# Transposing the last expert slot on TensorE, and spreading the next block's sums and squares over successive steps

## What is computed

```python
# experts: top 2 of 8, N=3072 tokens, D=384, F=1024
h = np.maximum(x[mask] @ w1[e], 0.0)
out[mask] += top2_w[mask, k, None] * (h @ w2[e])
# output network, d_ff=1536
rms = np.sqrt(np.mean(x * x, axis=-1, keepdims=True) + 1e-06)
xn = x / rms * rms_g
g = xn @ w_gate
silu = g * (1.0 / (1.0 + np.exp(-g)))
return (silu * (xn @ w_val) @ w_out)
```

## Time and profile before

| What | us |
|---|---|
| median of three runs | 1308.37 |
| the profiled execution | 1309.53 |
| its span, first to last instruction | 1307.8 |
| attention, up to about | 300 |
| experts, up to the last output matmul | 814.4 |
| first matmul of the output network | 832.5 |
| PE busy | 1244.2 (95%) |
| DVE busy | 858.9 (66%) |
| ACT busy | 458.4 (35%) |

### The profile page before, as it was taken

One profiled execution on the slowest core, in us unless ns is written; L12 is line 12 of the kernel. 1 busy time (PEld: TensorE's weight loads), 2 busy tenths in 40 slices (PEclk: granted clock), 3 DMA queues, 4 the chain that ended last, 5 costly groups with the idle time before them and its releaser, 6 DMA issues.

```text
span 1307.8 us, 26515 instructions
## 1 busy us (share of the span) xinstructions
PE 1244.2 (95%) x8915; PEld 1143.2 (87%) x8916; DVE 858.9 (66%) x1941; ACT 458.4 (35%) x982; POOL 444.2 (34%) x374
## 2 busy tenths in 40 slices
PE   4999999999899999999999998699999999999998
PEld 4777878777789989899998987599999999999997
DVE  7898888876578778787877876344454444444433
ACT  3565665654232222223222222233232323233221
POOL 8467777734641606061455530311010101010000
PEclk9999999999999999999999999699999999999999
DMA  5233433245413222232314310211010101010000
GB/s 214 87 97 127 131 124 119 65 165 224 145 50 133 84 99 99 85 113 73 132 48 161 140 43 25 73 37 37 19 55 1 55 19 37 19 36 18 0 19 19
DMA packets 36175, 105.46 MB, mean 81 GB/s; under 512 B 4992, under 2 KB 20352, under 8 KB 33664
## 3 DMA queue, kind: packets, MB, share of 16 engines
q1 hardware_dynamic: 27504, 56.41, 12.9%
q0 software_dynamic: 8592, 47.98, 10.3%
HBM read 77.83 MB, written 26.54 MB: 80 GB/s over the span
## 4 chain that ended last, share of the span: by engine, by line
PE 75%; DVE 7%; POOL 6%; issue 5%; ACT 5%; DMA 2%; another core or an unknown queue 0%; DVEq 0%; SPq 0%; ACTq 0%; POOLq 0%
PE pD L1776 12%; PE pD L1885 9%; PE pA L1885 9%; PE pA L1808 9%; PE pS L1808 8%; PE pA L1899 6%; PE pA L1584 5%; PE pA L1776 5%; PE pS L1899 3%; PE pA L1790 2%; PE pX L1749 1%; POOL qk L583 1%; DVE W L1087 1%; POOL prods L599 1%; DMA stage<-w 1%
## 5 line engine op out<-in xcount | busy, mean ns | idle before, releaser
L1520 DVE TENSOR_TENSOR gs<-pD,sig 128x384 f32<-128x384 f32 x96 | 53.5, 557 | 200.3 <-ACT sig L1022 200.3
L1263 DVE STREAM_TRANSPOSE pA<-pD 32x128 f32<-32x128 f32 x416 | 138.1, 332 | 54.6 <-PE pD L1776 48.9
L751 POOL DMA_INDIRECT pair<-y_sorted,y_row x48 | 46.5, 968 | 342.9 <-DVE z L1499 272.5
L1263 DVE STREAM_TRANSPOSE pA<-pA 32x128 f32<-32x128 f32 x400 | 132.8, 332 | 43.6 <-PE pA L1776 38.0
L926 ACT ACTIVATE hidH<-pA 128x512 fp32r<-128x512 f32 x110 | 65.8, 600 | 254.5 <-DVE pA L1263 244.9
L1584 PE MATMUL pA<-W 64*128 64x128 f32 (+3 forms) x1920 | 138.0, 284 | 16.3 <-DVE W L1087 13.0
L1776 PE MATMUL pD<-we,xsH 128*128 x462 | 145.6, 396 | 0.0
L1584 PEld LDWEIGHTS pA<-W 64*128 64x128 f32 (+3 forms) x1920 | 113.8, 171 | 35.5 <-DVE W L1087 18.7
L1022 ACT ACTIVATE sig<-pD 128x384 f32<-128x384 f32 x96 | 47.1, 491 | 211.2 <-PE pA L1885 211.1
L1808 PE MATMUL pA<-we,hidH 128*128 (+1 forms) x464 | 120.9, 342 | 0.0
L1087 DVE TENSOR_TENSOR W<-W,prods 128x512 f32<-128x512 f32 (+1 forms) x120 | 102.7, 862 | 20.9 <-PE pA L1584 17.1
(11 more groups left out here) (262 smaller groups left out, 2875.2 us busy)
## 6 DMA issues: line engine op xcount, KB each, us to landing
stage<-w POOLq DMA_DIRECT2D x14, 1536.0 KB
qk<-qk_t SPq DMA_DIRECT2D x24, 512.0 KB, 3.8
xs<-x_sorted SPq DMA_DIRECT2D x55, 192.0 KB, 2.4
y_sorted<-yo SPq DMA_DIRECT2D x55, 192.0 KB, 1.9
fT<-f_t SPq DMA_DIRECT2D x12, 512.0 KB, 5.7
vN<-v_n SPq DMA_DIRECT2D x24, 256.0 KB, 2.6
out<-fin SPq DMA_DIRECT2D x8, 576.0 KB, 2.8
stage<-w SPq DMA_DIRECT2D x2, 1536.0 KB
```

Source lines behind the costliest of these rows:

```text
L751: pool.indirect_dma_start(out=pair[:, j, k], out_offset=None, in_=y_sorted[:, :], in_offset=bass.IndirectOffsetOnAxis(ap=y_row[:, t * TS + ...
L1263: ins = dve.transpose(by_32[1][32 * q:32 * (q + 1), :, i], by_32[0][32 * i:32 * (i + 1), :, q])
L1520: dve.tensor_tensor(gs[:], pD[:, f % 2 * 512:f % 2 * 512 + TT], sig[f % 2][:], ALU.mult).then_inc(s_u, 1)
```

## The change

Two parts that have nothing to do with each other.

The last slot (`last_slot(t)`, t = 54): ACT rectifies both halves, PE transposes both (lines 1790 and 1795), and DVE's 16 transposes fall away. ACT's rectifying of the second half waits for the end of hidden(54), and PE's transposes wait for both rectified halves.

The output stage: `combine` becomes one call for each tile, at f = 2, 3 and 4, with its own semaphore steps; the squares are taken one tile each at f = 3, 4 and 5; the root stands at f = 6 alone; `norm` moves from f = 6 to f = 7. Semaphore `s_z` now counts 8 a block and `s_ms` 4. POOL's gathers wait for the third tile's sum.

```diff
+        def last_slot(t):
+            return t.i is None and t.c == SLOTS - 1
-        ZS, ZS_PAIR = 5, 2
+        ZS, MS = 8, 4
@@ POOL
-                    pool.wait_ge(s_z, (t - 2) * ZS + ZS_PAIR)
+                    pool.wait_ge(s_z, (t - 2) * ZS + 2 * TS)
@@ ACT rectify
-                if early(t):
+                if last_slot(t):
+                    act.wait_ge(s_ht, SLOTS - 1)
+                if early(t) or last_slot(t):
                     act.wait_ge(s_g1, t.times(2, 2))
                     ins = act.activation(hid[:, HF:], hidden_bank(t, 1), ACT.Relu)
@@ ACT
-            def mean_square(t):
+            def square_of(t, j):
+                act.wait_ge(s_z, t.times(ZS, 2 * j + 2 - ZS))
+                act.activation(square[j][:], z[:, j], ACT.Square, accum_out=ms[:, j:j + 1]).then_inc(s_ms, 1)
+            def root(t):
+                act.wait_ge(s_ms, t.times(MS, TS - MS))
                 if t.c >= 2:
-                    act.wait_ge(s_z, t.times(ZS, -2 - ZS))
+                    act.wait_ge(s_z, t.times(ZS, -1 - ZS))
                 act.activation(rms[:], ms[:], ACT.Sqrt, scale=1.0 / DM, bias=eps[:]).then_inc(s_ms, 1)
@@ ACT wide
-                    if f == 4 and (t + 1).before(NT2):
-                        mean_square(t + 1)
+                    if NEXT_SUM < f <= NEXT_SUM + TS and (t + 1).before(NT2):
+                        square_of(t + 1, f - NEXT_SUM - 1)
+                    if f == NEXT_SUM + TS + 1 and (t + 1).before(NT2):
+                        root(t + 1)
@@ DVE turn_hidden
+                if last_slot(t):
+                    return
@@ DVE
-            def combine(t):
-                for s in s_pair:
-                    dve.wait_ge(s, t.times(32, 32))
+            def combine(t, j):
+                dve.wait_ge(s_pair[j], t.times(32, 32))
@@ DVE wide
-                    if f == 3 and more:
-                        combine(t + 1)
-                    if f == 6 and more:
+                    if NEXT_SUM <= f < NEXT_SUM + TS and more:
+                        combine(t + 1, f - NEXT_SUM)
+                    if f == NEXT_Z - 1 and more:
                         norm(t + 1)
@@ PE turn_hidden
-                    pe.wait_ge(s_hl, t.times(2, 0 if early(t) else -1))
+                    pe.wait_ge(s_hl, t.times(2, 0 if early(t) or last_slot(t) else -1))
-                if early(t):
+                if early(t) or last_slot(t):
                     for k in range(FC // 2):
```

More of the change, by code:

```diff
@@ L460, in clear_rows @@
                 eng.dma_start(x_sorted[bass.ds(n + e * REGION, P), :], zero[:]).then_inc(s_zero, 16)
-        NEXT_Z = 8
+        NEXT_SUM, NEXT_Z = 2, 8
         TAB_COUNT, TAB = 1, 16
-        ZS, ZS_PAIR = 5, 2
+        ZS, MS = 8, 4
         FIRST_SUM, FIRST_NORM = (2, 4, 8), (6, 10, 12)
@@ L998, in first_mean_square @@
                                bias=eps[:]).then_inc(s_rms, 1)
-            def mean_square(t):
-                act.wait_ge(s_z, t.times(ZS, ZS_PAIR - ZS))
-                if t.c >= 2:
-                    act.wait_ge(s_z, t.times(ZS, -2 - ZS))
[L1005 to L1008, removed]
+            def square_of(t, j):
[3 more added lines that the diff above has]
+                act.wait_ge(s_ms, t.times(MS, TS - MS))
+                if t.c >= 2:
+                    act.wait_ge(s_z, t.times(ZS, -1 - ZS))
                 act.activation(rms[:], ms[:], ACT.Sqrt, scale=1.0 / DM, bias=eps[:]).then_inc(s_ms, 1)
@@ L1485, in first_norm @@
                 dve.tensor_scalar(z[:, j], z[:, j], inv[:, j:j + 1], None, ALU.mult).then_inc(s_first, 1)
-            def combine(t):
-                for s in s_pair:
-                    dve.wait_ge(s, t.times(32, 32))
[L1491 to L1501, removed]
+            def combine(t, j):
+                dve.wait_ge(s_pair[j], t.times(32, 32))
+                if j == 0:
+                    dve.wait_ge(s_tz, t.times(KC))
+                sh = share[:, bass.ds(t.times(TS, j), 1)]
+                dve.tensor_scalar(z[:, j], pair[:, j, 0], sh[:, 0, 0:1], None, ALU.mult).then_inc(s_z, 1)
+                dve.wait_ge(s_z, t.times(ZS, 2 * j + 1 - ZS))
+                dve.scalar_tensor_tensor(out=z[:, j], in0=pair[:, j, 1], scalar=sh[:, 0, 1:2], in1=z[:, j],
+                                         op0=ALU.mult, op1=ALU.add).then_inc(s_z, 1)
             def norm(t):
-                dve.wait_ge(s_ms, t.times(2))
+                dve.wait_ge(s_ms, t.times(MS))
                 dve.reciprocal(inv[:], rms[:]).then_inc(s_z, 1)
-                dve.wait_ge(s_z, t.times(ZS, 3 - ZS))
+                dve.wait_ge(s_z, t.times(ZS, 2 * TS + 1 - ZS))
                 for j in range(TS):
                     ins = dve.tensor_scalar(z[:, j], z[:, j], inv[:, j:j + 1], None, ALU.mult)
-                ins.then_inc(s_z, 2)
+                ins.then_inc(s_z, 1)
             def low_z(t, k):
```

## The result

The changed kernel takes 1302.0 us, the median of 9 runs from 1300.65 to 1305.37; the kernel before, 9 runs beside it, 1308.37 (1305.15 to 1309.28). The ratio over all these runs, which is not that of the two medians (0.9951), is 0.9964 with a 95% interval of 0.9951 to 0.9977. Two more comparisons in later sessions gave 0.9954 (0.9941 to 0.9968) and 0.9954 (0.9940 to 0.9967). So the change makes the kernel 0.4 to 0.5% faster, some 5 to 6 us. The kernel before took between 1303.7 and 1308.4 us in the four sessions, the last three of them on three different chips, so whole times are set side by side only within a session.

A forecast was written before the change was run, and what follows sets the result against it. PE was taken to bound the output stage, and the path through output(54) everything up to the output network. 1309.53 - 2.4 - 4.4 = 1302.7 us, less 0.4 for the median: 1302.3, between 1300.3 and 1304.3 (1300.0 to 1305.3 with rivals).

The forecast's parts named there:

- part 1: Last slot: output(54) starts 0.80 us earlier and runs at full clock, saving 1.58 more; -2.4 us in all.
- part 2: Output stage: seven stops of PE for `uL` fall away, with their refill and restart; -4.4 us.
- Seven stops: Output stage: PE's waits for `uL`, 2.6 us idle together plus 0.16 and 0.10 each, all to go; -4.4 us.
- the sigmoid of step 6 starts at T + 3.84: Output stage, T being the start of its gate_value: the sigmoid starts at T + 3.84 instead of T + 3.46, 0.38 late.
- the 1.2 us to spare: Output stage: margin left before PE stops, with the sigmoid of step 6 0.38 us late against 1.60 allowed.
- the allowance of 1.60: Output stage: a sigmoid may start 1.60 us late before PE feels it, from 2.22 less 0.62.
- the way to output(53): Last slot: stop of 0.69 us and transposes of 0.50 and 0.35 put output(53)'s first matmul at 803.32, 1.35 us later.
- the clock's 1.58 us: Last slot: output(54) took 5.66 us at the lower clock against 4.08 for output(53); 1.58 us to be saved.
- Rival 1: Last slot: the clock falls all the same, costing 1.58 us again; 1304.3 us, chance 0.12.
- Rival 2: Output stage: half its stops stay, from a longer table exchange or sums that push a product; 1304.9 us, chance 0.10.
- Rival 4: Either part does hardly anything, as the stop moves on to something unseen; 1305 to 1308 us, chance 0.08.
- Rival 3: Output stage: table exchange takes 5.46 us, the sigmoid of step 6 is 2.94 late, PE stops; 1312.8 us, chance 0.04.

The follow-up runs named there:

- experiment 3: Changed kernel with an extra, unread root and sigmoid of 128x3 ahead of the root; 1320.0 us, against 1301.87 of the changed kernel beside it.
- experiment 2: Changed kernel with the three sums and the three squares each all at once again, only the root apart; 1298.02 us, 0.9960 of the kernel before.
- experiment 5: Changed kernel with the last slot's second half transposed behind output(53), halves signalled singly; 1297.27 and 1299.07 us, 0.9954 and 0.9956 of the kernel before.
- part 1 alone: Kernel before with only the last slot changed, output stage as before; 1303.19 and 1306.65 us in two sessions, 0.9997 and 0.9993 of the kernel before.

## Why the prediction was right, point by point

**The total.** 1302.3 was forecast, 1302.0 measured. That they lie so close is in part luck: the nine runs of the changed kernel lie 4.7 us apart, the last 0.4 us of the forecast were a guess, and part 1 was put too high and part 2 a little too low. The sum was made for the profiled execution, and 6.8 us were to go from it; 7.3 went from the span behind the first matmul of the experts. The medians fell by 6.4, 6.0 and 6.6 us in three comparisons, the ratios say 4.7 to 6.

**Part 2: right in size, wrong in one step.** Seven stops were to go and went; 4.4 us were expected and 4.7 came, the 5.07 of the table above less 0.4 for the earlier rise of the clock. The method, idle time plus a fixed term for each stop, held in experiment 3 too; the term was 0.26 to 0.31 us by the lengths of the blocks, where I took 0.26. Wrong for four of the seven blocks was the step "the sigmoid of step 6 starts at T + 3.84". I took the 2.90 us of the earlier trace rows as a block that can be moved. In the three written-out blocks it can, and the sigmoid starts at T + 3.78. In the loop it can't: in the kernel before gate_value had ended long before the second load, so its wait cost nothing and was not seen; once the exchange comes earlier, the load waits for gate_value and starts only then, and the sigmoid at T + 4.74. Of the 1.2 us to spare, 0.3 were left there (1.60 - 1.28). The cover of `norm` was smaller as well: it ended at 1039.49 and PE's transposes stood at 1040.22, 0.7 us instead of 1.4. The forecast survived because the allowance of 1.60 was right, as experiment 3 shows. That the tile-by-tile spreading wins nothing I had not asked (experiment 2).

**Part 1: mechanism right, size too large.** Against the execution with a fallen clock 2.4 us were expected and 2.06 came. The mis-sized term is the way to output(53): 2.18 us after the last matmul of hidden(54) instead of 1.94. The stop was 0.75 us and not 0.69, the second four transposes took 0.55 up to the next matmul, not the 0.35 of the earlier trace rows, and the 48 matmuls 0.1 more than expected. So output(54) started 0.34 us later behind hidden(54) than the sum has it, just outside the 0.3 that the prediction allowed itself. The 0.2 us of the transposes are in the trace. Ahead of output(53) PE's sequencer (PEldq) reads which expert the slot has (`weights_of`, line 1762) and works out the address of the first weights (line 1814). Columns: how many, duration in ns three times, start, start again:

```profile
L1762 PEldq TENSOR_LOAD <-slot_i x1: 302/302/302, 800.6 to 800.6; - x1
L1814 PEldq FUSED_REGOPS  x1: 113/113/113, 801.5 to 801.5; - x1
```

That starts only when the stop has ended, at 800.6, and ends at 801.6; the first matmul of output(53) starts at 801.66. The fourth slot, from which the 0.35 was taken, has no such read, as its weights are fixed (`early(t)`). Before the change the read ran from 800.42 to 801.39, under matmuls of hidden(54). In experiment 5, where PE does not stop, the same four transposes took 0.35 again (801.68 to 802.03). The larger error is that I subtracted the clock's 1.58 us in full and then held it to be in the sum already. That is right for the profiled execution, but the median of the kernel before need not hold it, and part 1 alone brought 0.5 and 1.2 us, neither clear of no change.

**The rivals.** Rival 1, the clock falling in the last slot all the same, came in none of eight profiles. Rival 2 did not come, but was nearer than thought: in the loop blocks the exchange did become longer, by 0.9 us, and 0.3 us and not 1.2 stood between the changed kernel and new stops. Rival 4 did not come as a whole, though for part 1 alone the times can't rule it out. Rival 3 did not come: the loads end 0.02 us ahead of what follows them, in experiment 3 as in the changed kernel. The figure of the Trainium skill's page ScalarE: Activation LUTs (What ACT_TABLE_LOAD costs), 2.66 us for a switch, is twice what any run here shows (1.30 with the 0.02). Its mechanism, a late sigmoid that stops PE, is the one that experiment 3 made.

**A reading that was too bold.** From one trace of the sixth slot I took that 2.8 us of idle time and transposes leave the clock alone. Over 13 profiles it fell there in three. So a trace in which it doesn't fall proves little. Stops without transposes of 1.7 to 2.0 us, shorter than that stretch, were followed by a fall in 6 of 10 cases (2 of 3 in the last slot, 4 of 7 in experiment 3, which are not independent), the longer stretch with its transposes in 3 of 13. Another stop ahead of transposes, of 1.5 to 1.7 us near 318 us, was followed by none in the six profiles that have it. This speaks against the rule that transposes do not count (the Trainium skill, TensorE: Matmul & The Clock Gate, Part 4), but no experiment here was made for it.

## What to carry to other kernels

A stop of the busy engine costs its idle time, the pipeline's refill (0.26 to 0.31 us here) and perhaps a stretch at the lower clock (1.3 to 1.7 us here; the shortest stop with a fall behind it was 1.74 us, and stops of 0.75 us had none in eight profiles): judge it over several profiles, not one. When a block of instructions is moved, look for waits inside it that were free at the old place; in the loop here the table load stood behind the wait of the function that needs it, in the written-out blocks it did not. When a cost is taken from another place in the kernel, look for what that place leaves out, as the fourth slot leaves out the reading of its expert. And ask which single piece of a lump is too long: here it was the table exchange beside the squares, and splitting the rest won nothing.

## What the runs showed that I had not expected

The granted clock behind the same stop of the same program differs from execution to execution: behind 1.98 us it fell in two profiles of three, behind 1.82 us in three of 13. With the rise at the start of the output network, which came 3.0 to 5.6 us after it, this can make some 4.5 us of spread between runs of one kernel (1.6 and 1.6 for the two falls, 1.3 for the rise), not much less than the gain of this change. The timed runs agree: of 18 runs of the kernel before on one chip the six with a mean granted clock of 0.993 took 1305.7 to 1307.0 us, the twelve with 0.991 or 0.992 took 1307.3 to 1310.3. That mean does not tell a fall from a late rise. In some sessions all profiles also had a stop of 1.5 to 1.7 us at about 318 us, in the others one of 0.36, with 1.7 us between them in the expert stage (508.5 against 506.85 us up to hidden(54)). Why is not settled; the last three sessions had a chip each, so that chip and session can't be told apart.
